# Products of the first MLP in units of 512 columns, and two small steps of the recurrence over four column groups of TensorE

## Chip, cores, metric

One NeuronCore of one Trainium2 chip. The metric is the device time of one launch in microseconds (us).

## What is computed

For each of 4 batches x 8 heads the reference runs a recurrence over 768 tokens with a state of 48x48, and two MLPs over the 3072 rows that come out of it:

```python
k_n = k / (norm(k) + 1e-06)
for t in range(S):
    y[:, :, t] = q_t @ state
    state = state + beta_t * outer(k_t, v_t - state @ k_t)
x = y as (3072, 384)
h = ((x @ w1) * (x @ w2)) @ w3 @ w_out        # w1, w2: 384x1024, w3: 1024x1024, w_out: 1024x384
g = h @ w_in                                   # 3072x1024
solu = g * exp(g - max) / (sum exp(g - max) + 1e-9)
out = layer_norm(solu) * g_ln @ moe2_w_out     # 3072x384
```

## The kernel before, in words

The tokens are taken in 6 groups of 128 (`n`), each group in two halves (`tt`) of 64 tokens for the four batches. A half has two tiles (`g`, a pair of batches each) with 8 heads; the two batches of a pair (`bb`) stand in the upper and the lower 64 partitions.

*The chain of a half.* `k_state` (keys times state, L1412), `right_hand` (VectorE), `apply_inverse` (L1429), `keep_u` (ScalarE), `cross_half` (L1441), `right_hand2` (VectorE), `apply_inverse` again, `keep_u`, then for each tile `outputs` (L1455) and `add_state` (L1466), then `transpose_y` (L1480), `high_x` (ScalarE) and `low_x` (VectorE), which leave the outputs as two fp32r parts, `xh` and `xl`. All of the chain's matmuls up to the transposes are fp32, and each is two instructions on TensorE. `k_state` and `outputs` put 64 rows of output at a time, with a stationary operand of 64 columns; `apply_inverse` and `cross_half` already work in four places of 32 rows and 32 columns.

*The solve.* During group n VectorE makes the triangular inverse that group n + 1 needs: `system_rows`, `coefficients`, `substitute`, `eights_...`, `below_first`, `below_second`, `stationary`. They stand in one hand-written order with the chain's own VectorE steps, and each engine works strictly in its order.

*The filler.* Between the steps of the chain TensorE has 8 slots in each half (`fill(tt, slot)`). In group 0 they hold pieces of w3 @ w_out (`w3_wout`, L1509; `FILLS` says how many in which slot) and, in the second half, units of the first MLP; from group 1 on every slot holds a unit. A unit (`up`, L1496) is x @ w1 and x @ w2 for 128 of the 1024 columns and 256 tokens: 2 x 9 matmuls of 128x128 by 256 columns into the two halves of one PSUM bank. There are 12 halves x 8 = 96 units: 7 in group 0, 16 in each of groups 1 to 5, and 9 behind the last group. ScalarE copies the first product (`keep_a`, L1278), VectorE multiplies it with the second (`multiply`, L1086) into `msb`, and pairs of products are sent to `m_dram`. The unit in slot (0, 0) of a group is the last one of an older half, so that the slot behind it is the first that waits for the last `low_x` of the group before.

*Behind it.* `down` (L502) multiplies m with w3 @ w_out in matmuls of 512 columns, with m loaded back from `m_dram` in units (`load_unit`) and split by `early_high` and `early_low` while the last `up` units run; then come the second MLP's `hidden`, `turn` and `project`. The first loads of m and w34 are issued ahead of the last group's sends (`early_loads`).

## Time and profile before

| | us |
|---|---|
| median of 3 runs | 754.29 |
| lowest, highest | 753.59, 759.48 |
| the profiled execution | 754.57 |
| its span in the trace | 752.9 |
| TensorE busy | 739.8 (98%) |
| VectorE busy | 453.9 (60%) |
| ScalarE busy | 340.5 (45%) |
| mean granted TensorE clock, share of full speed | 0.998 |

The profiled execution took 1.67 us more than its span, which is what lies around the span, and 0.28 us more than the median. Times in the views are us from the span's start. A busy TensorE is not one at its peak, since records of pipelined matmuls overlap: what counts is the distance from start to start.

### The profile page before, as it was taken

The page shows a single profiled execution, that of the slowest core. Times are in us where ns is not written, and L with a number is a line of the kernel's source. Part 1 is how long each engine was busy: PE and PEld are TensorE (multiplying, and loading weights), DVE is VectorE, ACT ScalarE, POOL GpSimd, SP SyncE. Part 2 cuts the span into 40 slices and gives each one's busy share as a digit, 9 for nine tenths or more (in the row PEclk, how much of TensorE's full clock was granted, in tenths as well). Part 3 has the DMA queues.
Part 4 walks back from the last instruction along what each step waited for, and adds up shares of the span by engine and source line. Part 5 has one row for each costly group of instructions (what it writes and reads, how often), then busy time and mean ns, then how long its engine had stood idle before and what let it go on. Part 6 is the DMA issues. An engine that isn't in the chain of part 4 may idle for free.

```text
span 752.9 us, 22433 instructions
## 1 busy us (share of the span) xinstructions
PE 739.8 (98%) x9652; PEld 666.0 (88%) x9652; DVE 453.9 (60%) x759; ACT 340.5 (45%) x704; POOL 60.7 (8%) x97
## 2 busy tenths in 40 slices
PE   7999999999999999999999999999999999999997
PEld 5666999999999989999999988888899999999987
DVE  2956966874893885688131644443466666666663
ACT  5376445237336324623424444333444444444443
POOL 2343100100200010020000000000000000000000
PEclk9999999999999999999999999999999999999999
DMA  9970350350243025031114566610000000000001
GB/s 291 342 233 14 121 181 31 91 172 31 74 138 96 31 83 181 30 108 44 44 44 137 160 223 185 191 51 1 11 22 22 21 21 21 21 21 21 22 22 31
DMA packets 39815, 67.47 MB, mean 90 GB/s; under 512 B 4144, under 2 KB 27824, under 8 KB 39728
## 3 DMA queue, kind: packets, MB, share of 16 engines
q1 hardware_dynamic: 36640, 61.36, 26.5%
q10 hardware_dynamic: 3088, 4.82, 1.8%
q8 instruction: 71, 1.16, 0.7%
q14 instruction: 16, 0.13, 0.1%
HBM read 47.29 MB, written 18.87 MB: 88 GB/s over the span
## 4 chain that ended last, share of the span: by engine, by line
PE 96%; DMA 1%; DVE 1%; issue 1%; ACT 0%; ACTq 0%
PE ps L1496 29%; PE ps L538 13%; PE ps L502 13%; PE ps L515 13%; PE ps L1509 6%; PE ps L1455 3%; PE ps L1378 3%; PE ps L1412 3%; PE ps L1370 3%; PE ps L527 3%; PE ps L1466 3%; PE ps L1429 3%; PE ps L1441 1%; DMA vs<-in_wo 1%; PE ps L1480 1%
## 5 line engine op out<-in xcount | busy, mean ns | idle before, releaser
L1278 ACT COPY asb<-ps 128x256 f32<-128x256 f32 x96 | 35.8, 373 | 151.8 <-PE ps L1496 151.3
L1086 DVE TENSOR_TENSOR msb<-asb,ps 128x256 f32<-128x256 f32 x88 | 36.6, 416 | 96.0 <-ACT asb L1278 95.7
L538 PE MATMUL ps<-woh,uth 128*128 128x384 f32 x192 | 64.7, 337 | 0.5 <-DVE utl L455 0.5
L538 PE MATMUL ps<-woh,utl 128*128 128x384 f32 x192 | 64.5, 336 | 0.0
L538 PE MATMUL ps<-wol,uth 128*128 128x384 f32 x192 | 64.3, 335 | 0.0
L455 DVE TENSOR_TENSOR utl<-ps,uth 128x512 fp32r<-128x512 f32 x48 | 31.1, 686 | 47.9 <-ACT uth L343 47.9
L329 ACT ACTIVATE e<-ps,stats 128x1024 f32<-128x1024 f32 x24 | 26.8, 1117 | 67.6 <-DVE stats L421 67.6
L1496 PE MATMUL ps<-xh,w1h 128*128 128x256 f32 x288 | 56.9, 306 | 0.0
L502 PE MATMUL ps<-mh,w34h 128*128 128x512 f32 x144 | 56.0, 389 | 0.0
L502 PE MATMUL ps<-ml,w34h 128*128 128x512 f32 x144 | 56.0, 389 | 0.0
L502 PE MATMUL ps<-mh,w34l 128*128 128x512 f32 x144 | 56.0, 389 | 0.0
L1496 PE MATMUL ps<-xh,w2h 128*128 128x256 f32 x288 | 50.2, 283 | 0.0
L1496 PE MATMUL ps<-xl,w2h 128*128 128x256 f32 x288 | 50.2, 283 | 0.0
L1496 PE MATMUL ps<-xh,w1l 128*128 128x256 f32 x288 | 50.1, 283 | 0.0
L1496 PE MATMUL ps<-xl,w1h 128*128 128x256 f32 x288 | 50.0, 282 | 0.0
L1496 PE MATMUL ps<-xh,w2l 128*128 128x256 f32 x288 | 50.0, 282 | 0.0
L1236 ACT COPY us<-ps 64x768 f32<-64x768 f32 x46 | 36.5, 794 | 27.1 <-PE ps L1429 26.7
L427 DVE SCALAR_TENSOR_TENSOR mfirst<-ps,e 128x1024 f32<-128x1024 f32 x24 | 29.4, 1225 | 31.8 <-ACT e L329 31.8
L289 POOL TENSOR_TENSOR stats<-stats,half 128x1 f32<-128x1 f32 x24 | 13.2, 549 | 387.7 <-DVE stats L449 387.7
L1496 PEld LDWEIGHTS ps<-xh,w1h 128*128 128x128 f32 x288 | 40.4, 189 | 3.6
L515 PE MATMUL ps<-wih,hh 128*128 128x512 f32 x144 | 43.0, 407 | 0.0
L1496 PEld LDWEIGHTS ps<-xl,w2h 128*128 128x128 f32 x288 | 41.5, 192 | 0.0
(164 smaller groups left out, 1630.5 us busy)
## 6 DMA issues: line engine op xcount, KB each, us to landing
m_dram<-msb SPq DMA_DIRECT2D x42, 256.0 KB, 2.5
mrest<-m_dram SPq DMA_DIRECT2D x36, 256.0 KB, 6.0
kt<-in_keys SPq DMA_DIRECT2D x10, 512.0 KB, 6.2
vs<-in_vtok SPq DMA_DIRECT2D x6, 768.0 KB, 8.1
ks<-in_ktok SPq DMA_DIRECT2D x6, 768.0 KB, 4.7
out<-wst SPq DMA_DIRECT2D x48, 96.0 KB, 2.1
z<-in_queries SPq DMA_DIRECT2D x12, 256.0 KB, 7.4
mfirst<-m_dram SPq DMA_DIRECT2D x12, 256.0 KB, 5.2
```

Source lines behind the costliest of these rows:

```text
L329: act.activation(e[:, :], hb[s], ACT.Exp, bias=nmax[:, s:s + 1], accum_out=es[:, s:s + 1]).then_inc(expd, 1)
L427: dve.scalar_tensor_tensor(out=ubuf[:, s, :], in0=hb[s], scalar=1.0, in1=e[:, :], op0=ALU.mult, op1=ALU.mult, accum_out=us[:, s:s + 1]).th ...
L455: dve.tensor_tensor(utl[:, j, :, :], tb[j].rearrange("p (k c) -> p k c", c=P), uth[:, j, :, :].bitcast(F32), ALU.subtract).then_inc(ut_low, 1)
L502: ins = pe.matmul(hbank[par][k], w[:, f, k * P:(k + 1) * P], mm[:, u, f % UF, :, :].rearrange("p t c -> p (t c)"), start=(f == 0 and j == ...
L515: ins = pe.matmul(hb[slot % 2][:, c * 512:(c + 1) * 512], xx[:, slot, k, :], w[:, k, c * 512:(c + 1) * 512], start=(j == 0 and k == 0), st ...
L527: ins = pe.transpose(tb[j][:, k * P:(k + 1) * P], ubuf[:, s, c:c + P], ident[:, :])
L538: ins = pe.matmul(ob[s], xx[:, j, k, :], w[:, 4 * j + k, :], start=(j == 0 and k == 0 and p == 0), stop=(j == 1 and k == 3 and p == 2))
L1086: dve.tensor_tensor(stage(half, f)[:, f % 2, :], asb[:, f % 2, :], bbank[f % 2], ALU.mult).then_inc(product, 1)
L1236: ins = act.copy(us[u_rows(bb), :, bb, :], both[u_rows(bb)])
L1278: act.copy(asb[:, f % 2, :], abank[f % 2]).then_inc(a_kept, 1)
L1496: ins = pe.matmul(bank, w[:, k, cols], xx[:, par, k, :], start=(j == 0 and k == 0), stop=(j == 2 and k == KD - 1))
L1509: ins = pe.matmul(w34bank[f % 2], w3s[f][:, c, :], wos[c // 4][:, c % 4, :], start=(c == 0), stop=(c == KF - 1))
```

## The change

Three things are changed together.

1. A unit of `up` now takes all 512 tokens of a group for one `side` (w1 or w2): 9 matmuls of 512 columns into a bank of its own (`abank`, `bbank`, both single, as is `asb`). The number of these half units is again 96, with 16 in each of groups 1 to 5 and 16 behind the last group; group 0 has none. `xh` and `xl` exist twice, one pair for even and one for odd groups (`xhigh` lies where `mfirst` is later, `xlow` where `w3raw` was). A half unit's first side waits for `a_kept` of the one before, its second side for `product` of the one before. The unit in slot (0, 0) of group n is now the first one of group n - 1, and waits for the last `low_x` of that group. ScalarE copies in the even slots, VectorE multiplies in the odd ones, each time 512 columns.
2. `k_state` and `outputs` issue two matmuls where one was, each with 32 columns of the stationary operand, so that consecutive ones go to four groups of 32 output rows.
3. `FILLS` is laid out anew (4 pieces leave the first half of group 0 for the second), m goes to `m_dram` in one DMA per 512-column product, the loads of m and w34 start only after the last `low_x` and the last send of group 4, those of m's group 1 after the very last product, and the first load of w_out is split over two queues.

The diff, cut to its core:

```diff
+        with ExitStack() as shared:
+            mfirst = sb("mfirst", [P, 2, UF, 2, HT], F32, shared)
+        xhigh = sb("xhigh", [P, KD, GT], F32R)
+        sb("above_xhigh", [P, 4 * UF * HT - KD * GT])
...
+            sp.dma_start(unit(n % 2, u).rearrange("p f t c -> p f (t c)"),
+                         m_dram[n, :, UF * u:UF * (u + 1), :]).then_inc(mu_in[slot], 16)
...
-        def early_loads(sp):
-            for j in range(2):
-                sp.wait_ge(w34_sent[j], 16 * (KF // 2))
-            load_w34(sp, 0)
-            load_unit(sp, 0, 0)
-            load_unit(sp, 0, 1)
...
-            load_w34(sp, 1)
-            load_w34(sp, 2)
-            load_unit(sp, 0, 2)
-            load_w34(sp, 3)
-            load_unit(sp, 0, 3)
-            sp.wait_ge(product, KF * (2 * NG - 1) + 6)
+            for j in range(2):
+                sp.wait_ge(w34_sent[j], 16 * (KF // 2))
+            for u in range(NU):
+                load_w34(sp, u)
+                load_unit(sp, 0, u)
+            sp.wait_ge(product, KF * NG)
...
-        xh, xl = buf("xh", [P, 2, KD, HT], F32R), buf("xl", [P, 2, KD, HT], F32R)
-        asb = buf("asb", [P, 2, HT])
-        msb = buf("msb", [P, 2, 2, HT])
+        xh, xl = buf("xh", [P, KD, GT], F32R), buf("xl", [P, KD, GT], F32R)
+        asb = buf("asb", [P, GT])
+        msb = buf("msb", [P, 2, GT])
...
-        abank = [ps[:, 4 + j, 0:HT] for j in range(2)]
-        bbank = [ps[:, 4 + j, HT:2 * HT] for j in range(2)]
+        abank, bbank = ps[:, 4, :], ps[:, 5, :]
         w34bank = [ps[:, 4 + j, 0:DM] for j in range(2)]
         sbank = [ps[:, 6 + g, 0:DM] for g in range(NP)]
         ybank = [ps[:, 2 + g, 0:DM] for g in range(NP)]
 
-        FILLS = {(0, 0): 6, (0, 1): 4, (0, 2): 3, (0, 3): 3, (0, 4): 2, (0, 5): 2, (0, 6): 1, (0, 7): 1, (1, 0): 2}
+        FILLS = {(0, 0): 2, (0, 1): 4, (0, 2): 2, (0, 3): 2, (0, 4): 3, (0, 5): 3, (0, 6): 1, (0, 7): 1,
+                 (1, 0): 2, (1, 1): 2, (1, 2): 1, (1, 3): 1}
...
         def unit(n, tt, slot):
 
-            return (2 * n + tt - 2, KF - 1) if slot == 0 else (2 * n + tt - 1, slot - 1)
-
-        def is_up(n, tt, slot):
-
-            return not static_below(n, 1) or (tt == 1 and slot > 0)
...
+            def send_m(n, f):
+
+                sp.wait_ge(product, KF * n + f + 1)
+                sp.dma_start(m_dram[n, :, f, :], stage(n, f)).then_inc(m_sent[f % 2], 16)
+
+            def group(n):
+
+                ahead = n + 2 < NG
+                if n > 0:
+                    for f in range(KF // 2):
+                        send_m(n - 1, f)
...
+            sp.dma_start(wos[0][:, 3:4, :], wo1[:, 3:4, :]).then_inc(wo1_in[0], 16)
...
+            def multiply(n, f):
+
+                i = KF * n + f
                 dve.wait_ge(a_kept, i + 1)
-
-                if half == 2 * NG - 1:
-                    pass
-                elif f % 2 == 0 and not static_below(half, 1) or f >= 4:
-                    dve.wait_ge(m_sent[f // 2 % 2], 16 * (2 * half + f // 4))
-                elif f == 0:
-                    dve.wait_ge(w_low, 2 * KF)
-                dve.tensor_tensor(stage(half, f)[:, f % 2, :], asb[:, f % 2, :], bbank[f % 2],
-                                  ALU.mult).then_inc(product, 1)
+                dve.wait_ge(b_done, i + 1)
+                if i >= 2 and (n < NG - 1 or f < 2 or f == KF - 1):
+                    dve.wait_ge(m_sent[f % 2], 16 * (i // 2))
+                dve.tensor_tensor(stage(n, f), asb[:, :], bbank, ALU.mult).then_inc(product, 1)
 
             def group(n, ahead):
 
...
-                    if is_up(n, tt, slot):
+                    if n > 0 and slot % 2 == 1:
                         multiply(*unit(n, tt, slot))
...
+            def keep_a(n, f):
+                i = KF * n + f
+                act.wait_ge(a_done, i + 1)
+                if i == 0:
+                    act.wait_ge(w_low, 2 * KF)
+                else:
+                    act.wait_ge(product, i)
+                act.copy(asb[:, :], abank).then_inc(a_kept, 1)
...
-                    for bb in range(2):
-                        r = state_rows(bb)
-                        ins = pe.matmul(chain[g][u_rows(bb), hc(h)], kt[r, par, tile, h, :], us[r, g, bb, hc(h)],
-                                        start=True, stop=True)
+                    for place in range(2):
+                        for bb in range(2):
+                            r, at = state_rows(bb), HB * place
+                            ins = pe.matmul(chain[g][64 * bb + at:64 * bb + at + HB, hc(h)],
+                                            kt[r, par, tile, h, at:at + HB], us[r, g, bb, hc(h)],
+                                            start=True, stop=True)
...
                         r = STACK[bb] if q >= NP else u_rows(bb)
-                        ins = pe.matmul(chain[g][u_rows(bb), hc(h)], z[r, par, bb, tile, h, :],
-                                        us[r, g, bb, hc(h)], start=True, stop=True)
+                        for place in range(2):
+                            at = HB * place
+                            ins = pe.matmul(chain[g][64 * bb + at:64 * bb + at + HB, hc(h)],
+                                            z[r, par, bb, tile, h, at:at + HB],
+                                            us[r, g, bb, hc(h)], start=True, stop=True)
...
+            def up(n, f, side):
+
+                i = KF * n + f
+                if f == 0 and side == 0:
+                    pe.wait_ge(x_low, TPG * (n + 1))
+                if static_below(n, 1):
+                    pe.wait_ge(w_low, 2 * f + side + 1)
+                if side == 0:
+                    if i >= 1:
+                        pe.wait_ge(a_kept, i)
+                    bank, wh, wl, done = abank, w1h, w1l, a_done
+                else:
+                    if i >= 1:
+                        pe.wait_ge(product, i)
+                    bank, wh, wl, done = bbank, w2h, w2l, b_done
+                xhn, xln = xhs[n % 2], xls[n % 2]
                 cols = slice(f * P, (f + 1) * P)
-                for bank, wh, wl in ((abank[f % 2], w1h, w1l), (bbank[f % 2], w2h, w2l)):
-                    for j, (w, xx) in enumerate(((wh, xh), (wh, xl), (wl, xh))):
-                        for k in range(KD):
-                            ins = pe.matmul(bank, w[:, k, cols], xx[:, par, k, :],
-                                            start=(j == 0 and k == 0), stop=(j == 2 and k == KD - 1))
-                ins.then_inc(ab_done, 1)
+                for j, (w, xx) in enumerate(((wh, xhn), (wh, xln), (wl, xhn))):
+                    for k in range(KD):
+                        ins = pe.matmul(bank, w[:, k, cols], xx[:, k, :],
+                                        start=(j == 0 and k == 0), stop=(j == 2 and k == KD - 1))
+                ins.then_inc(done, 1)
...
-            up(2 * NG - 2, 0, KF - 1)
             for f in range(KF):
-                up(2 * NG - 1, 1, f)
+                for side in range(2):
+                    up(NG - 1, f, side)
 
```

## Rows read from the trace of the kernel before

**Rows 1.** The page: busy time by engine, and the chain that ended last

```profile
PE 739.8 (98%) x9652; PEld 666.0 (88%) x9652; DVE 453.9 (60%) x759; ACT 340.5 (45%) x704; POOL 60.7 (8%) x97
...
PE 96%; DMA 1%; DVE 1%; issue 1%; ACT 0%; ACTq 0%
```

**Rows 2.** TensorE's timeline where `up` ends: start, length, line, matmuls

```profile
425.60 0.52 PE L1496 MATMUL ps<-xh,w1h 128*128 128x256 f32 x3
...
427.76 0.40 PE L502 MATMUL ps<-mh,w34h 128*128 128x512 f32 x1
...
428.46 0.40 PE L502 MATMUL ps<-mh,w34h 128*128 128x512 f32 x1
...
430.51 0.39 PE L502 MATMUL ps<-mh,w34h 128*128 128x512 f32 x1
```

**Rows 3.** TensorE's timeline in group 4, chain and filler

```profile
302.93 0.62 PE L1496 MATMUL ps<-xh,w1h 128*128 128x256 f32 x3
...
305.28 1.15 PE L1370 MATMUL ps<-kt 48*64 48x64 f32 x32
...
310.72 0.88 PE L1429 MATMUL ps<-rr,ti 32*32 32x48 f32 x64
311.53 0.62 PE L1496 MATMUL ps<-xh,w1h 128*128 128x256 f32 x3
...
313.88 1.14 PE L1455 MATMUL ps<-us,z 112*64 112x48 f32 x32
314.95 0.92 PE L1466 MATMUL ps<-us,ks 64*48 64x48 f32 x32
...
325.02 2.07 PE L1412 MATMUL ps<-us,kt 48*64 48x48 f32 x64
327.02 0.62 PE L1496 MATMUL ps<-xh,w1h 128*128 128x256 f32 x3
```

**Rows 4.** The page's groups: VectorE over 512 columns of PSUM, mean ns

```profile
L455 DVE TENSOR_TENSOR utl<-ps,uth 128x512 fp32r<-128x512 f32 x48 | 31.1, 686 | 47.9 <-ACT uth L343 47.9
```

**Rows 5.** VectorE's timeline in the second half of group 0

```profile
74.42 0.95 DVE L1059 TENSOR_TENSOR rr<-vs,ps 128x768 f32<-128x768 f32 x1 [0.22 <-issue]
...
81.80 0.42 DVE L1086 TENSOR_TENSOR msb<-asb,ps 128x256 f32<-128x256 f32 x1
82.14 0.95 DVE L1066 TENSOR_TENSOR rr<-rr,ps 128x768 f32<-128x768 f32 x1
...
100.30 1.01 DVE L1072 TENSOR_TENSOR xl<-ps,xh 128x384 fp32r<-128x384 f32 x2
...
103.87 0.95 DVE L1059 TENSOR_TENSOR rr<-vs,ps 128x768 f32<-128x768 f32 x1
```

**Rows 6.** TensorE's timeline at the start and in group 0

```profile
11.17 4.51 PE L1509 MATMUL ps<-vs,kt 128*128 128x384 f32 x8 [2.16 <-DMA vs<-in_wo]
15.52 2.74 PE L1509 MATMUL ps<-vs,z 128*128 128x384 f32 x8
...
42.82 2.74 PE L1509 MATMUL ps<-vs,w3raw 128*128 128x384 f32 x8
45.40 1.45 PE L1509 MATMUL ps<-mfirst,w3raw 128*128 128x384 f32 x4
...
104.99 2.18 PE L1370 MATMUL ps<-kt 48*64 48x64 f32 x64
107.10 0.88 PE L1429 MATMUL ps<-rr,ti 32*32 32x48 f32 x64
```

**Rows 7.** Windows at the start: PE busy, granted clock, DMA share, GB/s

```profile
10.50:11.00 0.50, 0.00 (x0) 1.00 0.96 379
...
13.00:14.00 1.00, 1.00 (x3) 0.50 1.01 399
...
15.50:16.00 0.50, 0.50 (x3) 1.00 1.03 164
```

**Rows 8.** VectorE's timeline at the end of group 4

```profile
352.25 1.01 DVE L1072 TENSOR_TENSOR xl<-ps,xh 128x384 fp32r<-128x384 f32 x2
```

**Rows 9.** TensorE's timeline at the start of group 5

```profile
354.16 2.07 PE L1412 MATMUL ps<-us,kt 48*64 48x48 f32 x64
```

More of the change, by code:

```diff
@@ L195, in unit @@
         def unit(par, u):
-            slot = NU * par + u
-            return mfirst[:, slot, :, :, :] if slot < 2 else mrest[:, slot - 2, :, :, :]
+            at = ((0, 1, 2, 5), (3, 4, 6, 7))[par][u]
+            return mrest[:, at, :, :, :] if at < MU - 2 else mfirst[:, at - MU + 2, :, :, :]
         def steps(engine, tiles):
@@ L308, in high_m @@
             def high_m(n, uses, par, u):
-                act.wait_ge(mu_in[NU * par + u], 32 * uses)
+                act.wait_ge(mu_in[NU * par + u], 16 * uses)
                 if n >= 1:
@@ L374, in scalar @@
                     for j in range(2):
[L375 removed]
+                        act.wait_ge(m_sent[j], 16 * (KF // 2) * NG)
                     high_h(0, 0)
@@ L714, in unit @@
         def unit(n, tt, slot):
-            return (2 * n + tt - 2, KF - 1) if slot == 0 else (2 * n + tt - 1, slot - 1)
-        def is_up(n, tt, slot):
-            return not static_below(n, 1) or (tt == 1 and slot > 0)
+            return n - 1, (KF * tt + slot) // 2
         def three(view):
@@ L727, in attention_programs, with stage @@
         raw += [wfirst[:, j, :, :] for j in range(8)]
-        raw += [three(asb[:, :, :].rearrange("p a c -> p (a c)")[:, 0:DM]),
+        raw += [three(asb[:, 0:DM]),
                 three(mfirst.rearrange("p a f t c -> p (a f t c)")[:, KF // 2 * DM:KF // 2 * DM + DM])]
-        raw += [three(msb[:, :, :, :].rearrange("p a b c -> p (a b c)")[:, j * DM:(j + 1) * DM]) for j in range(2)]
-        def stage(half, f):
-            if half == 2 * NG - 1:
-                t = (us[:, :, 1, :], us[:, :, 0, :], rr[:, :, :], ysb[:, :, :])[f // 2]
-                return t[:, :, 0:HT]
-            return msb[:, f // 2 % 2, :, :]
+        raw += [three(msb[:, :, :].rearrange("p a c -> p (a c)")[:, j * DM:(j + 1) * DM]) for j in range(2)]
+        own = [us[:, :, :, :].rearrange("p g b n -> p (g b n)")[:, GT * j:GT * (j + 1)] for j in range(3)]
+        own += [t[:, :, :].rearrange("p g n -> p (g n)")[:, 0:GT] for t in (rr, ysb)]
+        def stage(n, f):
+            return own[f - 2] if n == NG - 1 and 2 <= f < KF - 1 else msb[:, f % 2, :]
         pieces = []
@@ L854, in sync @@
             load_v(1)
-            for n in range(1, NG):
-                if n == NG - 1:
-                    early_loads(sp)
-                group(n, n < NG - 1)
-            for f in range(0, KF // 2, 2):
-                send_m(2 * NG - 2, f)
+            for n in range(NG):
+                group(n)
         def gpsimd(pool):
@@ L1271, in keep_w34, with send_m @@
                 act.dma_start(w34_dram[:, f, :], w34s[:, f % 2, :]).then_inc(w34_sent[f % 2], 16)
-            def keep_a(half, f):
-                i = KF * half + f
-                act.wait_ge(ab_done, i + 1)
-                if not static_below(i, 2):
-                    act.wait_ge(product, i - 1)
-                act.copy(asb[:, f % 2, :], abank[f % 2]).then_inc(a_kept, 1)
-            def send_m(half, f):
-                act.wait_ge(product, KF * half + f + 2)
-                act.dma_start(m_dram[half, :, f:f + 2, :], stage(half, f)).then_inc(m_sent[f // 2 % 2], 16)
+            def keep_a(n, f):
[6 more added lines that the diff above has]
+                act.copy(asb[:, :], abank).then_inc(a_kept, 1)
+            def send_m(n, f):
+                act.wait_ge(product, KF * n + f + 1)
+                act.dma_start(m_dram[n, :, f, :], stage(n, f)).then_inc(m_sent[f % 2], 16)
             def group(n, ahead):
@@ L1291, in a_of @@
                     def a_of(slot, tt=tt):
-                        if is_up(n, tt, slot):
+                        if n > 0 and slot % 2 == 0:
                             keep_a(*unit(n, tt, slot))
@@ L1518, in fill @@
                 def fill(tt, slot, pieces=slice(None)):
-                    if is_up(n, tt, slot):
-                        half, f = unit(n, tt, slot)
-                        up(half, 1 - tt if slot else tt, f)
+                    if n > 0:
+                        up(*unit(n, tt, slot), slot % 2)
                     if n == 0:
```

103 lines of the change are left out of this document (42 added, 61 removed).

## Prediction

> **What bounds the kernel now.** I read the page first, then TensorE's timeline, then the other engines' only where TensorE could wait for them. The page says that TensorE is busy for 98% of the span and holds 96% of the chain that ended last [rows 1]. So time is won where TensorE's instructions come closer together, and lost where it must stand still. Busy time overlaps, so I take every price from start to start.
>
> **Part 1, units of 512 columns.** Eighteen matmuls of 256 columns take 427.76 - 425.60 = 2.16 us; nine of 512 columns in `down` take 430.51 - 428.46 = 2.05 us [rows 2]. The operands are of the same kind, fp32r and 128x128, so I take 2.05 for a half unit: 0.11 us less a slot. Between chain steps a unit takes 2.35 us (302.93 to 305.28, and 311.53 to 313.88 [rows 3]), that is 0.19 more for going in and out of the filler; the new one has to pay that as well, so it drops out.
>
> The other engines: the new copies and products have 512 columns. A VectorE operation of that width on PSUM takes 0.69 us [rows 4], against two of 0.42 [rows 5]. Banks and `asb` are single now, but the first side waits for a copy made a slot earlier and the second side for a product that VectorE can do during a first side of 2.05 us. I cost these waits at nothing; the cover is that 2.05 us against 0.69.
>
> **Part 2, where the filler went.** This is the part that costs. Before, 8 of the 96 units are done when group 1's first `apply_inverse` starts at 107.10 [rows 6]; afterwards 1 of 96 is. So 88 units are left before and 95 half units after: 88 x 2.16 = 190.1 against 95 x 2.05 = 194.8 us, **+4.7**.
>
> In return TensorE gets to that point earlier, but only as far as VectorE lets it. In the second half of group 0 VectorE works without a break from `right_hand` at 74.42 to the `right_hand` of group 1 at 103.87: it is the solve for group 1, with the two last `low_x` at 100.30 to 101.31 [rows 5]. The new first half unit waits for exactly these. What moves them:
> - Five multiplies stand ahead of them, each taking 82.14 - 81.80 = 0.34 us of VectorE's order [rows 5]; they are gone: -1.7.
> - `FILLS` takes 4 pieces out ahead of the chain of group 0. Eight instructions are 4 pieces and take 45.40 - 42.82 = 2.58 us [rows 6]. TensorE's later waits for ScalarE's copies, and pieces moved to slots (0, 4) and (0, 5), take some back. I take -2.2, between 0 and -2.6.
>
> So `low_x` ends at 101.31 - 1.7 - 2.2 = 97.4. TensorE will have done all that it had before that by about 90, an estimate: without the units its own work of that half is some 14 us at the rates of [rows 3], and two copies of `keep_u` and VectorE's answers lie between. It stands still for some 7 us. Then follow one half unit with its entry (2.05 + 0.1) and the key grams (107.10 - 104.99 = 2.1 [rows 6]), and `apply_inverse` starts at 101.7 in place of 107.10: **-5.4**.
>
> The stand has a second price, the clock. At the start of the kernel TensorE stood still for 2.16 us ahead of 11.17 [rows 6], and the granted clock was 1.00 at 10.5 to 11 and 0.50, the 1.2 GHz level, at 13 to 14; it was back at 1.00, the 2.4 GHz level, at 15.5 [rows 7]. The eight instructions from 11.17 took 4.35 us, later ones like them 2.58 [rows 6]: 1.8 us lost. The new stand is longer, so the clock will probably be low from the first matmul behind it; if it stays low for those 4.3 us, half of them is lost: **+2.2**, with 0 and 3.5 as ends.
>
> Sum of part 2: +4.7 - 5.4 + 2.2 = +1.5.
>
> **Part 3, 32 columns in four column groups.** Each call of `k_state` and of `outputs` goes from 32 instructions to 64. Two calls of `k_state` take 2.00 us now (325.02 to 327.02), one of `outputs` 1.07 (313.88 to 314.95) [rows 3]. The nearest row to the new form is `apply_inverse`: 64 instructions with 32 columns in four places, also 48 columns of moving data and fp32, in 311.53 - 310.72 = 0.81 us [rows 3], or 12.7 ns each. About 0.1 of that is the change of form (half of the 0.19), which a pair of `k_state` pays once: 2 x 0.71 + 0.1 = 1.52 against 2.00, -0.24 a call; `outputs` 0.81 against 1.07, -0.26. Behind 107.10 stand 18 calls of `k_state` (two in group 1, four in each of groups 2 to 5) and 20 of `outputs`: 18 x 0.24 + 20 x 0.26 = **-9.5**. Those ahead of it lie in VectorE's shadow.
>
> What the trace does not show is four column groups with shared rows: `apply_inverse` uses four row groups too, `outputs` reads 112 or 128 rows each time. For it speaks that the two column groups of today do not mind: `outputs`, whose instructions share rows, needs (1.07 - 0.1) / 32 = 30 ns an instruction, `k_state`, whose neighbours lie in different rows, (2.00 - 0.1) / 64 = 30 ns [rows 3]. So I take the row of `apply_inverse`. The bad end is that only two run at a time: a column group of `apply_inverse` is held for 4 x 11.1 = 44 ns by an instruction, two at a time make 22 ns, and a call 64 x 0.022 + 0.1 = 1.5 us.
>
> The Trainium skill, page "TensorE: Matmul & The Clock Gate", Part 3, says that weight loads overlap with matmuls in flight only when the row group differs. The trace does not bear it out for two column groups (30 against 30 ns above). The same page of the Trainium skill, under "Wait — 56ns, not 53.3ns?", gives a floor of about 25 ns from start to start however small the matmul; the trace disagrees with it, with 12.7 ns in `apply_inverse`. By the floor a call would take, as an estimate from that page, 1.6 to 1.7 us, and the kernel would come out near 780.
>
> **What else is moved.** `keep_u` must still fit under slot 4, now 0.11 us shorter: TensorE goes from 313.88 into `outputs` without idle time [rows 3], so some of it is in hand, and if not, it is 0.1 for each of 10 halves. The new wait in slot (0, 0) for the last `low_x` matters in every group. Between groups 4 and 5 that `low_x` ended at 353.26 [rows 8], and TensorE came to the slot at 354.16 + 2.0 = 356.2 [rows 9]: 2.9 us in hand. From slot (0, 4) on TensorE gains 12 x 0.11 + 4 x 0.26 + 4 x 0.24 = 3.3 us on it; VectorE gains 0.7 on fewer multiplies, and the waits it now has for TensorE (over 2 us) shrink too. I come out at 2 us in hand, so nothing. The loads of m and w34 now start as the last 16 half units do, 33 us ahead of `down`, whose first reads are split one by one behind those units: nothing. If a load came so late that ScalarE blocked on it, `keep_a` behind it, and then TensorE, would wait. m's second group is asked for after the last product, with `down`'s first 72 matmuls, 72 x 0.228 = 16 us, as cover: nothing. If that were not enough, `down` would show idle time. The split load of w_out may start TensorE 0.3 earlier; not counted.
>
> **Sum.** Part 1 is in the 4.7. +1.5 - 9.5 = -8.0 us; the whole gain of wider units, 96 x 0.11 = 10.6, goes for the loss of filler in group 0. The profiled execution of 754.57 becomes 746.6, the median of 754.29, 0.28 lower, **746.3**.
>
> **The rivals.**
> - *Column groups do not run four at a time.* If for both calls: 18 x (1.5 - 1.0) + 20 x (1.5 - 1.07) = +17.6 in place of -9.5, so 754.3 + 1.5 + 17.6 = 773. If only for `outputs`, with shared rows: -4.3 + 8.6, so 760. It decides from about 14.5 ns an instruction, where a call costs what it costs now. By the skill's rule on row groups the same thing happens. For it: no row has the combination. Against: 30 and 30 ns. Together 0.17.
> - *The stand in group 0 is worse*: `FILLS` moves nothing (0 for 2.2), the clock costs 3.5, or a group's slot (0, 0) waits 1 us for `low_x` at each of four boundaries. 750 to 754. For it: VectorE has only some 2 us in hand. 0.20.
> - *The stand is milder*: the clock stays up, or VectorE finishes earlier for want of waits. 742 to 744. 0.15.
> - *As forecast*, 744 to 749: 0.48.
>
> **How the numbers follow.** About 7.5 us, 1%, is what a measurement of this kernel can tell from nothing, and the forecast lies just beyond it. Faster by over 1% are the milder case and most of the lower half of the forecast: 0.50; within 1% the rest of it, the worse stand and `outputs` alone: 0.41; slower by over 1% the whole of the first rival: 0.09. The range reaches from just below the milder case to 760, where `outputs` alone fails, with 773 left out (both calls, 0.09, and what lies beyond the other cases' edges).
>
> **What would show it.** `up` should have 864 matmuls of 128x512 some 0.228 us apart. `k_state` pairs should take 1.5 us and `outputs` 0.8. TensorE should be idle for about 7 us around 90 to 97, released by `low_x`, with a clock below 1.00 behind it, and no other stand above 0.5 us up to `down`. `up` should end near 420 in place of 427.8. If `outputs` takes 1.5 us, the first rival is right; if the idle time recurs in groups 2 to 5, the second.

## The result and the profile after

The changed kernel takes 764.25 us (median of 4 runs, 762.88 to 766.00); the kernel before, run beside it, 755.22 (median of 4, 753.59 to 759.48). The ratio is 1.0096, with a 95% interval of 1.0051 to 1.0142. The forecast was 746.3 with a range up to 760; neither its sign nor its range held.

The profiled execution took 764.46 us, its span is 762.7 and its mean granted clock 0.988, where before had 754.57, 752.9 and 0.998. All rows and counts of stands below come from one profiled execution of each kernel, the times and ratios from all its runs. The page, as in [rows 1]: busy time by engine, the DMA queue q8, which the page calls "instruction", the chain that ended last.

```profile
PE 732.3 (96%) x10260; PEld 610.1 (80%) x10260; DVE 448.2 (59%) x711; ACT 332.5 (44%) x656; POOL 59.6 (8%) x97
...
q8 instruction: 76, 1.25, 0.7%
...
PE 88%; DVE 8%; issue 3%; ACT 1%; DMA 1%; DVEq 0%
```

TensorE has 608 matmuls more and is busy 7.5 us less, in a span that is 9.8 longer. In the chain "issue" went from 1% to 3%, and VectorE from 1% to 8%. So the work itself did become shorter, and the time between its instructions grew. TensorE's timeline where `up` ends, as in [rows 2]:

```profile
402.05 0.84 PE L1497 MATMUL ps<-xh,w2h 128*128 128x512 f32 x3
...
404.09 0.86 PE L1497 MATMUL ps<-xhigh,w1h 128*128 128x512 f32 x3
...
429.25 0.86 PE L1497 MATMUL ps<-xhigh,w1h 128*128 128x512 f32 x3
...
431.34 0.86 PE L1497 MATMUL ps<-xhigh,w2h 128*128 128x512 f32 x3
...
437.63 0.39 PE L497 MATMUL ps<-mh,w34h 128*128 128x512 f32 x1
```

A half unit takes 404.09 - 402.05 = 2.04 us on `xh` and `xl`, and 431.34 - 429.25 = 2.09 on `xhigh` and `xlow`; 2.05 was forecast. But `up` ends at 437.63, not near 420. The same timeline in group 4, which answers to [rows 3]:

```profile
311.79 0.89 PE L1449 MATMUL ps<-us,z 112*32 112x48 f32 x64
312.61 0.92 PE L1461 MATMUL ps<-us,ks 64*48 64x48 f32 x32
313.46 0.54 PE L1449 MATMUL ps<-us,z 112*32 112x48 f32 x31
315.05 0.57 PE L1449 MATMUL ps<-us,z 128*32 128x48 f32 x33 [1.05 <-issue]
315.55 0.92 PE L1461 MATMUL ps<-us,ks 64*48 64x48 f32 x32
...
323.53 1.57 PE L1403 MATMUL ps<-us,kt 48*32 48x48 f32 x128
325.03 0.97 PE L1497 MATMUL ps<-xhigh,w1h 128*128 128x512 f32 x3
```

The first call of `outputs` takes 312.61 - 311.79 = 0.82 us and the pair of `k_state` 325.03 - 323.53 = 1.50, as priced (0.81 and 1.52). The second call of `outputs` is cut in two after 31 of its 64 instructions, and TensorE stands still for 1.05 us with nothing to wait for: no semaphore, only "issue". Such a place is called a stand here. The list of TensorE's waits adds these up (line, releaser: us in total, times, longest):

```profile
PE ps L1449 <- issue: 7.8, 5, 3.0
PE ps L1360 <- issue: 4.7, 2, 3.9
PE ps L1461 <- issue: 2.6, 2, 1.4
...
PE ps L1497 <- DVE xl L1068: 1.4, 1, 1.4
PE ps L1497 <- issue: 1.3, 1, 1.3
...
PE ps L1433 <- issue: 0.8, 1, 0.8
```

Group 0, TensorE's timeline, which answers to [rows 6]:

```profile
46.28 1.84 PE L1360 MATMUL ps<-kt 48*64 48x64 f32 x54
51.99 0.90 PE L1360 MATMUL ps<-kt 48*64 48x64 f32 x10 [3.87 <-issue]
...
91.91 0.74 PE L1449 MATMUL ps<-us,z 112*32 112x48 f32 x29
95.65 0.91 PE L1449 MATMUL ps<-us,z 128*32 128x48 f32 x35 [3.00 <-issue]
...
102.39 1.46 PE L1497 MATMUL ps<-xh,w1h 128*128 128x512 f32 x3 [1.44 <-DVE xl L1068]
...
106.23 2.08 PE L1360 MATMUL ps<-kt 48*64 48x64 f32 x64
108.25 0.88 PE L1421 MATMUL ps<-rr,ti 32*32 32x48 f32 x64
```

VectorE's timeline there, as in [rows 5]:

```profile
77.45 0.95 DVE L1055 TENSOR_TENSOR rr<-vs,ps 128x768 f32<-128x768 f32 x1 [1.03 <-issue]
...
101.31 1.02 DVE L1068 TENSOR_TENSOR xl<-ps,xh 128x384 fp32r<-128x384 f32 x2
```

And windows of the changed kernel (after the busy times: granted clock, DMA share, GB/s):

```profile
50.00:55.00 5.00, 3.01 (x14) 1.89 (x14) 0.00 (x0) 2.67 (x8) 1.94 (x2) 0.64 0.16 54
55.00:60.00 5.00, 5.00 (x102) 3.50 (x100) 0.95 (x1) 2.35 (x7) 0.00 (x0) 0.67 0.02 3
...
90.00:95.00 5.00, 2.65 (x88) 2.31 (x81) 4.92 (x5) 1.43 (x3) 2.77 (x1) 0.76 0.62 200
95.00:100.00 5.00, 4.35 (x133) 3.87 (x136) 4.90 (x4) 2.28 (x5) 0.00 (x0) 0.66 0.18 38
```

Behind the stands of 3.87 and 3.00 us the granted clock falls to its lower level, 1.2 GHz, for part of the time. Before had it at 1.00 from 40 to 110 us. From 107 us to `down` the changed kernel has it at 1.00 too.

The difference of the two spans, 9.8 us (9.9 by the finer rows), splits into three stretches:

| stretch | before | after | difference | forecast |
|---|---|---|---|---|
| to group 1's first `apply_inverse` | 107.10 | 108.25 | +1.2 | -3.2 |
| from there to `down` | 320.7 | 329.4 | +8.7 | -4.8 |
| from `down` to the end of the span | 325.1 | 325.1 | 0 | 0 |

The forecast of the first line is -5.4 + 2.2, that of the second +4.7 - 9.5. Behind 107 us (that is, later than 107 us) the gaps from start to start of TensorE's matmuls that are over 0.7 us and have no releaser but "issue" add up to 12.5 us, in 9 stands; before has 2.8 in 2. That is 9.7 of the 13.5 us by which the second line was missed.

### The profile page after: what moved, and what is told of

The parts are those of the page before. It is cut to its first block, busy times and chain, and to the rows that moved or that the text cites. A ratio compares the mean times of both kernels' runs of the same rounds, so it can differ in the third digit from the quotient of the medians.

```text
span 762.7 us, 23469 instructions
## 1 busy us (share of the span) xinstructions
PE 732.3 (96%) x10260; PEld 610.1 (80%) x10260; DVE 448.2 (59%) x711; ACT 332.5 (44%) x656; POOL 59.6 (8%) x97
## 3 DMA queue, kind: packets, MB, share of 16 engines
q8 instruction: 76, 1.25, 0.7%
## 4 chain that ended last, share of the span: by engine, by line
PE 88%; DVE 8%; issue 3%; ACT 1%; DMA 1%; DVEq 0%
PE ps L1497 28%; PE ps L533 13%; PE ps L497 13%; PE ps L510 13%; PE ps L1360 4%; PE ps L522 3%; PE ps L1461 3%; PE ps L1449 2%; PE ps L1368 2%; PE ps L1421 2%; PE ps L1403 2%; PE ps L1510 2%; PE ps L1433 1%; DVE tmp L1025 1%; PE ps L1475 1%
## 5 line engine op out<-in xcount | busy, mean ns | idle before, releaser
L1078 DVE TENSOR_TENSOR msb<-asb,ps 128x512 f32<-128x512 f32 x43 | 29.4, 685 | 100.4 <-PE ps L1497 91.6
L1271 ACT COPY asb<-ps 128x512 f32<-128x512 f32 x48 | 28.1, 586 | 122.7 <-PE ps L1497 117.8
L284 POOL TENSOR_TENSOR stats<-stats,half 128x1 f32<-128x1 f32 x24 | 13.2, 548 | 399.6 <-DVE stats L444 399.6
L510 PE MATMUL ps<-wih,hl 128*128 128x512 f32 x144 | 41.0, 392 | 0.0
L510 PE MATMUL ps<-wil,hh 128*128 128x512 f32 x144 | 40.9, 392 | 0.0
L1200 ACT COPY gd<-ps 32x256 f32<-32x256 f32 x96 | 34.8, 363 | 12.6 <-PE ps L1360 11.5
L533 PEld LDWEIGHTS ps<-woh,uth 128*128 128x128 f32 x192 | 36.1, 188 | 1.8 <-DVE utl L450 0.8
L1360 PEld LDWEIGHTS ps<-kt 48*64 48x64 f32 x768 | 27.4, 151 | 12.2 <-issue 11.6
L533 PEld LDWEIGHTS ps<-wol,uth 128*128 128x128 f32 x192 | 36.1, 188 | 0.9
L416 DVE TENSOR_REDUCE stats<-ps 128x1 f32<-128x1024 f32 x24 | 29.4, 1223 | 11.6 <-PE ps L510 10.2
L533 PEld LDWEIGHTS ps<-woh,utl 128*128 128x128 f32 x192 | 36.0, 188 | 0.0
```

Of the source, the lines that this page charges most:

```text
L416: dve.tensor_reduce(nmax[:, s:s + 1], hb[s], AX_X, ALU.max, negate=True).then_inc(maxed, 1)
L510: ins = pe.matmul(hb[slot % 2][:, c * 512:(c + 1) * 512], xx[:, slot, k, :], w[:, k, c * 512:(c + 1) * 512], start=(j == 0 and k == 0), st ...
L533: ins = pe.matmul(ob[s], xx[:, j, k, :], w[:, 4 * j + k, :], start=(j == 0 and k == 0 and p == 0), stop=(j == 1 and k == 3 and p == 2))
L1078: dve.tensor_tensor(stage(n, f), asb[:, :], bbank, ALU.mult).then_inc(product, 1)
L1200: ins = act.copy(gd[rows, tile * H:(tile + 1) * H, :], bank[rows, :, HB * place:HB * (place + 1)])
L1271: act.copy(asb[:, :], abank).then_inc(a_kept, 1)
```

## Experiments

*The theory.* TensorE stands still because its instructions are not there. What speaks for it is where the stands are. Count the matmuls from the start of the program: the stands of the changed kernel lie ahead of number 475, 1363 and 1488, and then 2247, 3129, 4398, 5158, 5538, 5793, 6045, 6553 and 7822. Number 1363 is a wait for ScalarE. The others are 126 to 127.5 or a multiple of that apart (2247 - 1488 = 6 x 126.5, 3129 - 2247 = 7 x 126, 4398 - 3129 = 10 x 126.9, 5158 - 4398 = 6 x 126.7). Each matmul has a weight load beside it in the records (PE and PEld, x10260 each), so 127 of them are 254 instructions. The queue q8 moved 76 packets, 1.25 MB, or 16.4 KB each; before it moved 71, for 608 matmuls less (608 x 2 / 254 = 4.8 packets):

```profile
q8 instruction: 71, 1.16, 0.7%
```

So a packet is some 254 instructions, and a stand comes where TensorE has used up one packet and the next isn't there. The packets' own times say the same. Of the 13 traces of this case ten have such stands over 0.7 us between 107 us and `down`, 62 in all, and each ends 1.1 to 1.9 us after a packet of q8 has landed.

The stand at 315.05, shown above, can be followed from end to end. TensorE's last 127 matmuls before it (64, 32 and 31) are one packet's worth; they begin at 311.79 and are through in 2 us. The next packet begins at 312.42, 0.6 us after TensorE entered the one before, lands at 313.77, and TensorE goes on 1.3 us later. The DMA view for 311 to 315 us has nothing else in it:

```profile
DMA packets 1, 0.02 MB, mean 4 GB/s; under 512 B 0, under 2 KB 0, under 8 KB 0
...
q8 instruction: 1, 0.02, 2.1%
```

So here the next packet starts only when TensorE is already in the last one it has, and TensorE gets to it 3.3 us after that entry, even with idle DMA engines. What TensorE does faster than that ends in a stand. Behind 107 us no packet begins less than 3.5 us after the one before it in this trace, and in none of the traces below less than 3.2.

The Trainium skill, page "Runtime: NRT & Kernel Launch", section "Instruction fetch mechanics", says that instructions come in blocks of 16 KiB, 256 instructions, which the sequencer fetches by a DMA queue of its own while the one before is executed. The trace agrees with that: 16.4 KB and some 254 instructions a packet. The page also says that the cost of crossing a block is mostly hidden; 12.5 us of stands disagree.

*The rivals.* Either the loss belongs to the wider units and to group 0 (the missing filler, the clock). Or calls over four column groups cost more among other work than `apply_inverse` does by itself. Two runs take the change apart.

**e1_units_only** is the changed kernel with `k_state` and `outputs` of before (the cut shows `k_state`; `outputs` likewise):

```diff
-                    for place in range(2):
-                        for bb in range(2):
-                            ... kt[r, par, tile, h, at:at + HB] ...
+                    for bb in range(2):
+                        ... kt[r, par, tile, h, :] ...
```

> The changed kernel with k_state and outputs back at 64 columns. Theory S (instruction supply): the 32-column calls save 9.5 us by their own rate, but their doubled instructions empty TensorE's supply of instructions and about 10 us of stands without a releaser come back in groups 1 to 5; then this kernel is within 2 us of the changed one, 762 to 766 where before is 755, its stands inside outputs, add_state and k_state in groups 1 to 5 sum to under 4 us (13 in the changed kernel), and its calls take 1.0 and 1.07 us. Rival P (the prices of the prediction hold, and the loss is all in group 0 and in the half units): about 9 us slower than the changed kernel, 772 to 775.

Measured: 759.94 us (10 runs) against 756.33, a ratio of 1.0037 (1.0015 to 1.0058). Behind 107 us there is no stand at all. In group 0 there are two for want of instructions, 3.6 us at matmul 475, in the key grams, and 1.2 in `add_state` at 93.39, and a wait of 3.46 for `xl`. The time lies between the two that were expected: below the 762 to 766 of the theory and far below the rival's 772 to 775.

**e2_cols_only** is the kernel before with 32 columns in both steps, and nothing else (the cut shows `outputs`; `k_state` likewise):

```diff
-                        ins = pe.matmul(chain[g][u_rows(bb), hc(h)], z[r, par, bb, tile, h, :],
-                                        us[r, g, bb, hc(h)], start=True, stop=True)
+                        for place in range(2):
+                            at = HB * place
+                            ins = pe.matmul(chain[g][64 * bb + at:64 * bb + at + HB, hc(h)],
+                                            z[r, par, bb, tile, h, at:at + HB],
+                                            us[r, g, bb, hc(h)], start=True, stop=True)
```

> The kernel before with only the two steps at 32 columns. Theory S: the calls take 0.81 and 0.75 us as in the changed kernel, but stands without a releaser appear beside them, 6 to 12 us in all, so the time is within 4 us of before. Rival P: no new stands, 9 to 11 us faster, about 745.

Measured: 769.15 against 756.33, ratio 1.0140 (1.0078 to 1.0202). The part that was to bring 9.5 us costs some 10.6 by the ratio, between 6 and 15. That is worse than the theory expected, which had it within 4 us of before. Behind 107 us 11 stands add up to 19.1 us, ahead of matmuls 1866, 2880, 3135, 3389, 4023 and so on, again multiples of 127 apart. The clock adds to it: at the stands that end at 112, 153, 179 and 312 us it fell to 0.50, the 1.2 GHz level, for 20 us in all, with TensorE busy. So the stands come with the number of instructions, not with the units, and the first rival can account for no more than e1 shows.

**e3_cols_spread** asks whether it is their density. It is e2 with slot 5 of the filler moved between the two tiles:

```diff
+                    fill(tt, 5)
                     outputs(n, par, tt, 1)
                     add_state(n, par, tt, 1)
-                    fill(tt, 5)
```

> The kernel before with the two steps at 32 columns and the filler of slot 5 moved between the two tiles' outputs and add_state, so that the longest dense block has 192 instruction pairs halved to 96. The work is the same. Theory S: the stands of e2 shrink to under half, and it is 2 to 6 us faster than e2. Rival P: no difference from e2 within 1 us, or slower, since the transposes come nearer to the copy of tile 1's outputs.

Measured: 767.74, ratio 1.0133 (1.0082 to 1.0185). It was expected 2 to 6 us faster than e2, and the ratios differ by far less than their intervals. But the stands are other ones: 6 with 16.5 us in place of 11 with 19.1. All six of e2 whose packet began within 1.5 us after TensorE entered the one before, 0.8 to 1.4 us each (3135, 4023, 4785, 6307, 7195 and 8592), are gone. Of the others 2880 and 6052 stayed as they were, 1866 and 6561 became longer, 3389 shorter, and one of 3.4 us at 5038 is new. TensorE's timeline of e3 at the last of them:

```profile
308.13 1.57 PE L1413 MATMUL ps<-us,kt 48*32 48x48 f32 x128
309.63 0.62 PE L1501 MATMUL ps<-xh,w1h 128*128 128x256 f32 x3
310.09 0.52 PE L1501 MATMUL ps<-xl,w1h 128*128 128x256 f32 x3
314.01 1.01 PE L1501 MATMUL ps<-xh,w1l 128*128 128x256 f32 x3 [3.41 <-issue]
```

It stands in the middle of a unit, where no semaphore is. The DMA view of e3 for 303 to 310 us (queue, kind: packets, MB, share of 16 engines):

```profile
q1 hardware_dynamic: 441, 1.87, 82.7%
```

and for 310 to 313 us:

```profile
q1 hardware_dynamic: 179, 0.78, 91.4%
q8 instruction: 1, 0.02, 3.0%
```

From 303 us on the DMA engines were full of the next group's loads, 2.6 MB that the kernel issues one right after the other when a group ends. TensorE entered its last packet, 127 matmuls ahead of the stand, at 308.2. In the changed kernel, at 312, the next one began 0.6 us after that; here it began 2.8 us after, at 311.05, and landed at 312.48. TensorE went on 1.5 us after that. The clock fell too; the windows of e3 there:

```profile
310.00:314.00 4.00, 0.61 (x6) 0.40 (x4) 1.50 (x3) 0.00 (x0) 0.00 (x0) 0.84 0.81 239
314.00:318.00 4.00, 3.99 (x33) 3.76 (x35) 0.42 (x1) 0.37 (x1) 0.00 (x0) 0.50 0.03 8
```

So there are two kinds of stand. In 31 of the 62 the packet begins on time, 0.4 to 1.5 us after TensorE entered the one before, with the DMA engines at most 25% busy until then. TensorE is through its 127 matmuls in 2.0 to 2.9 us, gets to the next ones 2.8 to 4.1 us after the entry, and stands for 0.7 to 1.7 us. `outputs` and `add_state` of both tiles are now 192 matmuls in some 3.3 us, 2.2 us a packet; before they were 128 in about 3.95, 3.9 us a packet, which was enough. In 26 the packet begins 2.1 to 6.0 us after the entry, beside DMA engines that are over 80% busy in that time; these stands are 0.9 to 4.3 us long. The other five have a packet on time and loads beside it.

**e4_old_fills** tests part 2's move of filler by itself: the changed kernel with the `FILLS` of before.

```diff
-        FILLS = {(0, 0): 2, (0, 1): 4, (0, 2): 2, (0, 3): 2, (0, 4): 3, (0, 5): 3, (0, 6): 1, (0, 7): 1,
-                 (1, 0): 2, (1, 1): 2, (1, 2): 1, (1, 3): 1}
+        FILLS = {(0, 0): 6, (0, 1): 4, (0, 2): 3, (0, 3): 3, (0, 4): 2, (0, 5): 2, (0, 6): 1, (0, 7): 1, (1, 0): 2}
```

> The changed kernel with the FILLS of before. Theory S: the stand of 3.9 us inside the key grams of group 0 at 48 comes from having little filler (4 pieces fewer) ahead of them while the loads are still running; with the old FILLS it is gone or under 1 us, and the clock is not at half speed from 51 to 58. The chain then starts 2.6 us later but runs on; the first apply_inverse of group 1 starts between 105 and 108 in place of 108.25, and the time is 0 to 3 us below the changed kernel. Rival: FILLS is worth what I priced, 2.2 us, and without it the kernel is 2 us slower.

Measured: 765.92, ratio 1.0128 (1.0058 to 1.0197), which can't be told from the changed kernel's 1.0096. It was expected 0 to 3 us below. Group 1's first `apply_inverse` starts at 105.97 in place of 108.25, as expected, but the stand at matmul 475 is still there, 2.1 us, and the one at 6045 grew from 1.0 to 3.2. The placement of the pieces is neither the cause nor a cure.

**e5_after_spaced** is the changed kernel with its bulk loads taken apart: each goes between two sends of m, where SP waits for a product in any case.

```diff
                     for f in range(KF // 2):
                         send_m(n - 1, f)
+                        if f == 1 and n + 1 < NG:
+                            load_v(n + 1)
...
-                    load_k(n + 2)
                     load_kq(n + 2, 1)
-                    load_v(n + 2)
-                if n > 0:
-                    for f in range(KF - 2, KF):
+                for f in range(KF - 2, KF):
+                    if n > 0:
                         send_m(n - 1, f)
+                    if f == KF - 2 and ahead:
+                        load_k(n + 2)
...
-            load_k(1)
             sp.wait_ge(w34_done, KF)
             load_v(1)
+            load_k(1)
```

> The changed kernel with its bulk loads taken apart: the next keys by token, values and keys by column, 2.8 MB that were issued in one go at a group's end, are issued one by one between sends, and the second group's keys by token wait until w3 @ w_out is done. The work and TensorE's order are the same. Theory S with the transfer of instructions queued behind bulk loads: the long stands (3.9 at 48, 3.0 at 92, those above 2 us elsewhere) go or shrink below 1.5 us, the clock drops at most twice, and the time is 3 to 7 us below the changed kernel, 757 to 761; the short ones of 1.0 to 1.7 us inside dense blocks stay. Rival (the stands come from the density of instructions alone): no change.

**e6_after_spaced_spread** is e5 with slot 5 spread as in e3.

> As e5, and with the filler of slot 5 between the two tiles' outputs and add_state. Theory S: the short stands inside outputs and add_state go too, 4 to 7 us less than e5, 752 to 756, level with or just below the kernel before. Rival: as e5.

**e7_cols_spaced_spread** is e3 (256 columns, 32-column steps, spread) with the loads taken apart in the same way.

> The kernel before with the two steps at 32 columns, slot 5 between the tiles, and the loads taken apart. Theory S: e3 had 17 us of stands behind 107, of which 14 in five of 2 us and more that lie within 10 us behind a burst of loads; those go, and with the clock staying up the time is 745 to 753, the best of all. Rival (32 columns do not pay whatever the supply): 760 or more.

**e8_before_spaced** is the kernel before with the loads taken apart, and nothing else: what that edit is worth without the dense steps.

> The kernel before with only its loads taken apart. Control for e7: the kernel before has two stands of 2.8 us in all, so at most 3 us faster; the same within 1% whatever the theory.

These four, with the kernel before beside them at 757.35:

| | us | ratio to before | 95% | stands behind 107 us |
|---|---|---|---|---|
| e5 | 757.36 | 1.0012 | 0.9981 to 1.0043 | 8.6 in 7 |
| e6 | 752.72 | 0.9940 | 0.9906 to 0.9974 | 4.5 in 3 |
| e7 | 748.31 | 0.9879 | 0.9816 to 0.9941 | 4.8 in 3 |
| e8 | 755.61 | 0.9970 | 0.9937 to 1.0002 | 3.4 in 2 |

Loads apart bring the changed kernel's ratio from 1.0096 to 1.0012, spreading slot 5 that to 0.9940; the intervals of neighbours don't overlap. Neither edit changes what is computed or how many instructions TensorE has. e8 says that the loads alone are worth 0.3% where the steps aren't dense, and 0.6% at the end of its interval. In e5 one expected thing failed: in group 0 a stand of 3.9 us is left at matmul 1488, where the packet began 5.6 us after TensorE entered the one before, beside full DMA engines, and one of 1.7 us at 3636. Long ones were to be gone or under 1.5. e7 is the fastest of all, faster than the kernel before and the changed one. Its three stands are in `cross_half`, 2.5 and 0.9, and in `k_state`, 1.5; none is in `outputs` or `add_state`. Its timeline in group 4, where the changed kernel stood:

```profile
311.80 0.89 PE L1461 MATMUL ps<-us,z 112*32 112x48 f32 x64
312.61 0.92 PE L1473 MATMUL ps<-us,ks 64*48 64x48 f32 x32
313.46 0.62 PE L1503 MATMUL ps<-xh,w1h 128*128 128x256 f32 x3
...
315.81 0.89 PE L1461 MATMUL ps<-us,z 112*32 112x48 f32 x64
316.63 0.92 PE L1473 MATMUL ps<-us,ks 64*48 64x48 f32 x32
```

The two calls of `outputs` take 0.81 and 0.82 us, with a unit between them. In e5 the stand in group 0's key grams, which begin at 46.28 in the changed kernel, went from 3.87 to

```profile
49.28 0.56 PE L1362 MATMUL ps<-kt 48*64 48x64 f32 x10 [1.13 <-issue]
```

and the granted clock from 50 to 60 us was 1.00 in both windows of five.

**e11_cols_spaced** is e7 without the spread, so that e2, e3, e7 and e11 make a square.

> As e7 (32 columns, loads taken apart) but with slot 5 back behind both tiles. Theory S: against e7 the short stands inside outputs and add_state come back, 4 to 7 us: 752 to 756. Against e2 the long ones behind bursts of loads are gone: 12 us less or more. If taking the loads apart did all of it, it equals e7.

Measured: 758.09, ratio 1.0007 (0.9973 to 1.0041), a little above the 752 to 756 expected. There are 11 stands with 13.2 us, the longest 2.2; e2's six short ones are all there, at the same matmuls. By the ratios the loads apart are worth 10 us from e2 to e11, and the spread another 10 from e11 to e7; the intervals don't overlap. Without the loads apart the spread was worth 0.5 us, from e2 to e3, which is nothing clear: there the late packets were left.

The stands and the clock account for the whole stretch from group 1's first `apply_inverse` to `down`. Take 317.9 us for the kernel before without its 2.8 us of stands, and 326.4 for the wide units (e1, e9 and e10, which have no stand there, take 326.1 to 326.6). Subtract the forecast 9.5 us where the steps have 32 columns, add the stands in the stretch, and half of the time that the trace shows at the 1.2 GHz level. The sum is an estimate; all is in us:

| | stands | time at 1.2 GHz | sum | measured |
|---|---|---|---|---|
| changed | 12.5 | 0 | 329.4 | 329.4 |
| e2 | 15.8 | 19.3 | 333.9 | 333.3 |
| e3 | 12.2 | 18.9 | 330.1 | 330.9 |
| e4 | 12.1 | 6.8 | 332.4 | 331.8 |
| e5 | 8.6 | 2.9 | 327.0 | 327.3 |
| e6 | 4.5 | 0 | 321.4 | 323.2 |
| e7 | 4.8 | 3.4 | 314.9 | 317.2 |
| e8 | 3.4 | 3.4 | 323.0 | 323.1 |
| e11 | 11.6 | 6.8 | 323.4 | 323.4 |

(In e2, e3 and e11 the first stand counted above lies ahead of the stretch.) Where slot 5 isn't spread the sum is within 0.6 us. The three kernels with slot 5 spread take 0.8 to 2.3 us more than it, which may be what the spread itself costs; no run shows that alone.

**e9_units_spaced** is e5 with the 64-column steps of before: parts 1 and 2 of the change alone, with the loads apart.

> The changed kernel with the two steps at 64 columns and the loads taken apart: the half units and the empty slots of group 0 alone, with few stands for want of instructions. By the prediction's prices for parts 1 and 2 it is 1.5 us slower than before; by e1 (2.8 us slower, with a stand of 3.8 us in group 0 that was a load's fault) 0 to 3 us. The stand ahead of the first half unit stays, released by low_x, with the clock at half speed behind it.

Measured: 758.67 against 756.79, ratio 1.0017 (0.9995 to 1.0038), or +1.3 us. Behind 107 us there is no stand. In group 0 there are still one of 1.5 us at matmul 475 and one of 2.4 in `add_state`, which ends at 90.51. TensorE's timeline:

```profile
97.44 1.65 PE L1494 MATMUL ps<-xh,w1h 128*128 128x512 f32 x3 [1.49 <-DVE xl L1070]
...
103.14 0.88 PE L1421 MATMUL ps<-rr,ti 32*32 32x48 f32 x64
```

and its windows:

```profile
92.00:96.00 4.00, 3.95 (x66) 3.49 (x64) 3.97 (x2) 0.75 (x2) 0.00 (x0) 0.50 0.97 282
96.00:100.00 4.00, 2.56 (x6) 2.07 (x7) 3.97 (x5) 0.00 (x0) 0.00 (x0) 0.50 0.44 162
```

**e10_units_warm** is e9 with 16 products of the identity, 32 instructions, into a bank that is free there, ahead of group 1's first half unit. Nothing reads them.

```diff
+                    if n == 1 and tt == 0:
+                        pe.wait_ge(w34_kept, KF)
+                        for _ in range(16):
+                            pe.matmul(ps[:, 5, 0:P], ident[:, :], ident[:, :], start=True, stop=True)
                     fill(tt, 0)
```

> As e9, with 16 matmuls of the identity (32 instructions) into an unused bank of PSUM ahead of the first half unit; what they compute is used by nobody. If the low clock behind the stand costs the 2.2 us I priced, this one is 1 to 2.5 us faster than e9 and the granted clock stays at or near 1.00 from the first half unit on. If these matmuls only run at the low clock themselves and the clock does not rise earlier, no difference, or slower by up to 1 us.

Measured: 755.64, ratio 0.9991 (0.9962 to 1.0020). That is 3.0 us below e9, but the intervals overlap, and the spans of the two profiled executions differ by 0.3 us the other way. The clock was 1.00 from 92 to 100 us, and 0.65 from 88 to 92, ahead of the new products, so these can't be what raised it. `apply_inverse` started at 103.51, no earlier than in e9: `low_x` ended 1.8 us later here. The price of the clock can be read all the same. From the first half unit to `apply_inverse` it takes 4.30 us at 1.00 (99.21 to 103.51 in e10), and 5.70 in e9 (97.44 to 103.14), where the clock was 0.50 until 100.5: 1.4 us.

## Why the prediction was wrong

**The step that failed** is part 3's sum, -9.5 us, with "no other stand above 0.5 us up to `down`" in the section on what would show it. It priced 38 calls by their own length and put the supply of twice the instructions in them at nothing. The lengths were right, 0.82 and 1.50 us for 0.81 and 1.52. But a packet's 127 matmuls now last only 2 to 2.5 us there, and the next one needs 3.2 to 4.1, more beside bulk loads. In the changed kernel that made 12.5 us of stands behind 107 us. By the ratios part 3 costs +10.6 us alone (e2) and +4.4 in the changed kernel, against e1. The price of a call was sound, as the sums of the table above say. With the loads apart and slot 5 spread the same 32 columns bring 748.31 against e8's 755.61, -7.3, with intervals that just touch, and e7 still has 1.4 us of stands more than e8. A hint stood in the trace of the kernel before, whose list of TensorE's waits has

```profile
PE ps L1441 <- issue: 2.4, 2, 1.6
```

These two stands, 2.8 us from start to start, lie behind 107 us in `cross_half`, which is as dense as the new steps, and both beside loads: for one the packet took 3.0 us where others take about 1, for the other it began 2.6 us after TensorE entered the one before.

**Part 1**: half units of 2.04 us held for `xh` and `xl`; those that read `xhigh` and `xlow` take 2.09, 48 x 0.05 = 2.4 us in all. That is the second share of the 13.5 by which the stretch to `down` was missed: 9.7 of stands, 2.4 of this, and 1.4 that no run places. It isn't the clock, which is 1.00 there, and it comes with the units: e1 and e9, which have neither stands there nor the 32-column steps, take 326.1 and 326.6, where 317.9 + 4.7 + 2.4 = 325.0 us would be. No wait for the banks or `asb`, single now, is to be seen.

**Part 2**: +4.7 isn't seen by itself, but e9, where it stands with the gain in group 0, gives +1.3 us for parts 1 and 2 against +1.5 forecast. That this fits is in part luck: e9 takes some 4 us more than forecast for the units, and lacks the 2.8 us of stands that before has. In e9 the last `low_x` ends where it was forecast, 97.4, and `apply_inverse` follows at 103.14, forecast 101.7 + 2.2 = 103.9. In the changed kernel `low_x` ended 4.9 us later than in e9. The stand of 3.87 us in the key grams holds up VectorE's first `right_hand` and all behind it: the second half's stood at 77.45, where 74.42 less 2.2 was forecast (in e9 it stood at 72.51), so the 2.2 us gained for `FILLS` became a loss of 3.0. This is the second step that failed, and it had the same cause. From there to the end of `low_x`, 102.33, it is 24.9 us, with 26.9 before ([rows 5]): 2.0 shorter, and 1.7 was forecast.

The idle time in group 0 was forecast at 7 us and is 1.44, in e9 1.49. TensorE came to it late: by a wait of 1.8 us for `keep_u` at 89, by the stand of 3.00, and at the lower clock (in e9 0.50 from 92 to 96 us). The prediction put the low clock behind that idle time; it was low ahead of it as well. Behind it the clock cost 1.4 us in e9 and 1.6 in the changed kernel (102.39 to 108.25, for 4.30 at 1.00), of the 2.2 priced.

**What was held to cost nothing** did, from group 1's first half unit on: TensorE is not idle for `low_x` in slot (0, 0) of groups 2 to 5, nor for `keep_u` under slot 4, nor in `down` for the loads that start later, and from `down` to the end both take 325.1 us.

**The rivals.** Column groups do run four at a time, with shared rows too, so the first rival's mechanism is wrong. That the measured 764 lies between its two times, 760 and 773, is chance. The second rival, a worse stand in group 0, is right in part: the 2.2 us for `FILLS` did not come, but what took them was the supply of instructions. In groups 2 to 5, where it also looked for idle time, nobody waits for `low_x`. No rival had the supply of instructions in it.

The Trainium skill, page "TensorE: Matmul & The Clock Gate", under "Wait — 56ns, not 53.3ns?", has the floor of about 25 ns by which the prediction reckoned some 780. It was rightly set aside: 64 instructions with shared rows take 0.82 us, 12.8 ns each.

**What stays open**: why half units on `xhigh` and `xlow` are 0.05 us slower, and where the other 1.4 us of the units go, which no run here took apart; whether the products of e10 gain anything; and how long a given packet waits beside loads. The kernel before and e2 are the same program up to matmul 475. In both the DMA engines were full when the packet was due; it began some 5 us after TensorE entered the one before, without a stand, in the kernel before, and some 8 us, with a stand of 2.8 us, in e2.

## What to carry over

Before you cut a matmul into smaller ones, count TensorE's instructions a microsecond over the whole dense stretch, not only the length of one call. Here a packet of some 127 matmuls needed about 3 to 4 us from the moment when TensorE entered the one before, so steps at 13 ns a matmul must be shorter than a packet and have long matmuls beside them. Look in the waits of TensorE for "issue" without a semaphore. Where such stands are a fixed number of instructions apart, the supply is the bound, and it can be eased by moving long work between the dense steps. Do not issue megabytes of loads at once beside dense work: here packets of instructions were late beside them, and taking the loads apart was worth 6 us (the changed kernel) and 10 us (e2) with dense steps, and 0.3% without.

## What was not expected of the hardware

- TensorE's instructions arrive in packets of 16.4 KB, one for some 127 matmuls with their weight loads, 3.2 us or more apart. A packet usually began only after TensorE had entered the one before; where it came too late, TensorE stood still, in the middle of a unit too, and went on 1.1 to 1.9 us after the packet had landed (e3: packet to 312.48, next matmul 314.01).
- Packets are late beside bulk traffic: in e3 one began 2.8 us after TensorE had entered the one before, where it is 0.6 in the changed kernel beside idle DMA engines; q1 took 82.7% of the 16 engines from 303 to 310 us and 91.4% from 310 to 313. A stand of 3.41 us followed.
- A stand costs twice when the granted clock falls behind it: 0.50 from 314 to 318 us in e3, with TensorE busy all the time. It fell for some 20 us in e2 and in e3; the nine stands of the changed kernel behind 107 us, the longest 1.7 us from start to start, left it at 1.00, while in e11 it fell at 108.8 us, behind one of 1.6.
- Two column groups, with shared or with different rows, took 30 ns an instruction of 64 columns; four took 12.8 ns an instruction of 32 columns in `outputs`, whose rows are shared, as against 12.7 in `apply_inverse`, whose rows differ.
